# Windowed attention with both key blocks joined before the exponential, and changed places of splits and output copies

## What is computed

```python
# 1: attention, 8 heads of 64, window of 128, a bias per head that falls with the distance
scores = 0.125 * q @ k.T - slope[h] * abs(t - s)    # where 0 <= t - s < 128, else -1e9
x = softmax(scores) @ v
# 2: gated layer with a spatial product over tokens
h = relu(x @ w_in); u, v = h[..., :512], h[..., 512:]
v = (v - mean(v)) / sqrt(var(v) + 1e-6)
x = (u * (w_spatial @ v + b_spatial)) @ w_out
# 3: four experts, each a causal attention with one head of 64; a token takes the best two of w_gate
out = sum(weight[e] * (causal_softmax(0.125 * (x @ wq[e]) @ (x @ wk[e]).T) @ (x @ wv[e]) @ wo[e]))
```

## Time and profile before

| | |
|---|---|
| median of 3 runs | 510.14 us (510.04 to 512.35) |
| the profiled execution | 509.63 us, its span 507.8 us |
| granted TensorE clock | 0.999 |
| busy: PE, PEld, DVE, ACT, POOL | 97%, 84%, 59%, 54%, 39% |
| transposes of stage 1 (L1284) | 256 |

### The profile page before, as it was taken

One profiled execution on the slowest core, in us unless ns is written; L12 is line 12 of the kernel. 1 busy time (PEld: TensorE's weight loads), 2 busy tenths in 40 slices (PEclk: granted clock), 3 DMA queues, 4 the chain that ended last, 5 costly groups with the idle time before them and its releaser, 6 DMA issues.

```text
span 507.8 us, 10924 instructions
## 1 busy us (share of the span) xinstructions
PE 492.6 (97%) x3981; PEld 425.1 (84%) x3981; DVE 301.7 (59%) x1124; ACT 275.9 (54%) x828; POOL 200.4 (39%) x376
## 2 busy tenths in 40 slices
PE   8899999999999999999999999999999999999997
PEld 5677998998776789999876789999876779999875
DVE  6986773566766743246766762246777664235683
ACT  6876472446577643245567754235567663235554
POOL 4665432212434533433334553251244454161331
PEclk9999999999999999999999999999999999999999
DMA  7948020013110240004111070002301000000111
GB/s 216 326 109 254 3 83 1 1 36 106 43 53 2 61 127 1 1 1 113 50 32 43 2 188 1 1 1 48 114 24 53 1 3 1 1 0 13 36 43 52
DMA packets 31785, 28.51 MB, mean 56 GB/s; under 512 B 5810, under 2 KB 24242, under 8 KB 31732
## 3 DMA queue, kind: packets, MB, share of 16 engines
q1 hardware_dynamic: 31732, 27.82, 18.8%
HBM read 20.74 MB, written 4.72 MB: 50 GB/s over the span
## 4 chain that ended last, share of the span: by engine, by line
PE 74%; DVE 14%; ACT 5%; issue 3%; POOL 2%; DMA 1%; SPq 0%; DVEq 0%; ACTq 0%; POOLq 0%
PE bank L1254 14%; PE bank L1255 13%; PE bank L1256 13%; PE bank L1241 7%; PE bank L1284 6%; PE bank L1324 5%; PE bank L1515 4%; PE bank L1493 4%; PE bank L1475 4%; ACT p L748 2%; DVE neg L1039 2%; DVE k_lo L1141 1%; PE bank L1260 1%; DVE ring L857 1%; DVE q L1136 1%
## 5 line engine op out<-in xcount | busy, mean ns | idle before, releaser
L484 POOL TENSOR_SCALAR ring<-ring,r 128x256 f32<-128x256 f32 (+2 forms) x144 | 67.9, 483 | 83.0 <-DVE r L868 82.6
L567 POOL TENSOR_SCALAR p<-p,r,wgt 128x128 f32<-128x128 f32 (+3 forms) x64 | 38.1, 607 | 97.6 <-DVE wgt_last L1085 42.4
L589 ACT ACTIVATE ring<-ring,neg 128x256 f32<-128x256 f32 (+2 forms) x144 | 67.9, 474 | 13.9 <-DVE neg L857 13.7
L748 ACT ACTIVATE p<-bank,neg 128x128 f32<-128x128 f32 (+4 forms) x72 | 39.1, 547 | 47.0 <-DVE neg L1039 46.9
L857 DVE CUSTOM_DVE_ANT_0 ring<-bank,bias 128x256 f32<-128x256 f32 (+1 forms) x128 | 43.9, 385 | 16.5 <-PE bank L1241 16.1
L532 POOL TENSOR_TENSOR g_lo<-uT,g_hi 128x288 fp32r<-128x288 f32 x32 | 27.2, 872 | 42.6 <-ACT g_hi L710 42.6
L1284 PE MATMUL bank<-ident,ring 128*128 128x128 f32 (+1 forms) x256 | 37.8, 282 | 4.7 <-POOL ring L484 4.7
L1241 PE MATMUL bank<-k,q 64*128 64x256 f32 (+2 forms) x320 | 38.7, 369 | 1.2 <-DVE neg L857 0.8
L1324 PEld LDWEIGHTS bank<-pt,v_in 128*64 128x64 f32 x576 | 28.2, 136 | 13.6 <-issue 11.3
L1284 PEld LDWEIGHTS bank<-ident,ring 128*128 128x128 f32 (+1 forms) x256 | 26.9, 138 | 14.8 <-POOL ring L484 7.7
L1254 PE MATMUL bank<-g_hi,w_c_hi 128*128 128x288 f32 x128 | 38.5, 301 | 0.6
(11 more groups left out here) (184 smaller groups left out, 1402.5 us busy)
## 6 DMA issues: line engine op xcount, KB each, us to landing
v_in<-v SPq DMA_DIRECT2D x16, 256.0 KB, 4.0
out<-o_sb SPq DMA_DIRECT2D x16, 256.0 KB, 2.0
q<-qT SPq DMA_DIRECT2D x15, 256.0 KB, 4.7
k<-kT SPq DMA_DIRECT2D x15, 256.0 KB, 5.7
w_in_raw<-w_in SPq DMA_DIRECT2D x4, 512.0 KB, 6.5
w_cat_raw<-wcat SPq DMA_DIRECT2D x1, 1544.0 KB, 7.8
w_spatial_raw<-wsT SPq DMA_DIRECT2D x1, 1152.0 KB, 9.9
k_hi<-k_hi SPq DMA_DIRECT2D x8, 144.0 KB, 2.5
```

The source lines that it names most:

```text
L484: last = nc.gpsimd.tensor_scalar(p, p, r1[:, i % 2, h:h + 1], 0.0, ALU.mult, ALU.add)
L567: nc.gpsimd.tensor_scalar(p, p, r3[:, i % 2, e:e + 1], by, ALU.mult, ALU.mult).then_inc(s3_sd, 1)
L589: nc.scalar.activation(x, x, ACT.Exp, bias=neg1[:, u % SLOTS1:u % SLOTS1 + 1], scale=-1.0, accum_out=sum1[:, i % 2, h:h + 1]).then_inc(s1_ ...
L748: nc.scalar.activation(p3[:, w % P3_SLOTS, 0:n], scored3(w), ACT.Exp, bias=neg3[:, w % 4:w % 4 + 1], scale=1.0, accum_out=sum3[:, i % 2, e ...
```

## The change

For every query row, a key column of the query's own block is allowed exactly where the same column of the block before is masked. After bias and mask, DVE takes the smaller of both (`join1`: the ring holds the negated scores), so that 128 columns remain for the exponential, the scaling and one transpose per head. The transposed probabilities of all four heads are copied by ACT. DVE then multiplies this copy by `diag`, ones where the key is not behind the query. The values are `pt` times v of the block before, plus the masked `pt` times (v of the own block minus v of the block before). POOL makes these differences (`v_steps`), four per sequence. The first tile stays as it was. `norm_v` of the first three tiles goes from DVE to POOL, vn has a place for every tile, and its splits (`high_vn`, `low_vn`) move behind the turns.

In stage 3 `low_qk(5)` goes ahead of `top2_b(0)`, `low_qk(7)` ahead of the maxima of units 6 and 7, `high_qk(6)` ahead of two exponentials, and the output copies of tiles with index 1 and 2 ahead of the exponentials of their turn.

```diff
+def slots1(g):
+    at = units1(g)[0][0] % SLOTS1
+    return slice(at, at + len(units1(g)))
...
+vn = sb("vn", [P, NT, DM], F32, at + 4 * NT * DM)
...
+v_step = sb("v_minus_v_of_tile_above", [P, NT - 1, H, D], F32)
+diag = sb("keys_up_to_query", [P, P], F32)
...
+def joined1(b, g):
+    return (NG1 - 4) * b + g - 3
+def columns1(g):
+    return 2 * P if G1[g][0] < NT - 1 else P
+def t1_bank(g):
+    return 2 + (g % 2 if G1[g][0] == 0 else g // 2 % 2)
...
+    nc.gpsimd.affine_select(out=diag[:], in_=diag[:], compare_op=ALU.is_ge, fill=0.0, base=0,
+                            pattern=[[1, P]], channel_multiplier=-1).then_inc(s_diag, 1)
+    def v_steps(b, t):
+        pool.wait_ge(s_v_in[t - 1], 16 * (b + 1))
+        pool.wait_ge(s_v_in[t], 16 * (b + 1))
+        if t == NT - 1:
+            pool.wait_ge(s_vz if b else s_vz0, b if b else 1)
+        nc.gpsimd.tensor_tensor(v_step[:, t - 1], v_in[:, t], v_in[:, t - 1], ALU.subtract).then_inc(s_vd, 1)
...
-            p = ring[:, u % SLOTS1, 0:w]
+            p = ring[:, u % SLOTS1, 0:P]
...
+        def norm_v(i):
+            pool.wait_ge(s1_rs, NT * b + i + 1)
+            nc.gpsimd.tensor_scalar(vn[:, ORDER1[i], :], v_sb[:, i % 2, :], mv[:, i % 2, 0:1], rstd[:, i % 2, :],
+                                    ALU.subtract, ALU.mult).then_inc(s1_vn, 1)
...
+            if first and m % 2 and m // 2 + 1 < NT:
+                v_steps(0, m // 2 + 1)
             if first and m in TABLES_AT:
                 tables(TABLES_AT.index(m), 2 * m + 5)
             for i in range(NT - 2):
                 if m == 2 * i + 4 + first:
                     rstd_of(i)
-                if m == 2 * i + 6 + first:
-                    low_vn(i, 0)
-                    low_vn(i, 1)
+                    norm_v(i)
         pool.wait_ge(s1_xl, NT * (b + 1))
         nc.gpsimd.tensor_copy(xs[:, :, 0:LAST], x_hi[:, :, S - LAST:S])
         nc.gpsimd.tensor_copy(xs[:, :, LAST:P], x_lo[:, :, S - LAST:S]).then_inc(s1_xs, 1)
-        rstd_of(NT - 2)
-        for i in range(NT - 3, NT - 1):
+        for i in range(NT - 1):
             low_vn(i, 0)
             low_vn(i, 1)
+            if i == 0:
+                rstd_of(NT - 2)
...
-        for w in range(U3):
+        for w in range(2 * E):
             scale3(w)
         if more:
-            for g in range(3):
-                scale1(b + 1, g)
+            for t in range(1, NT - 1):
+                v_steps(b + 1, t)
+        for w in range(2 * E, U3):
+            scale3(w)
+        if more:
+            v_steps(b + 1, NT - 1)
+            scale1(b + 1, 0)
+            scale1(b + 1, 1)
+            scale1(b + 1, 2)
...
+        if i:
+            act.wait_ge(s1_cb, joined1(b, g))
         for u, h in units1(g):
-            x = ring[:, u % SLOTS1, 0:w]
-            act.wait_ge(s1_bi, U1 * b + u + 1)
+            x = ring[:, u % SLOTS1, 0:P]
+            if i == 0:
+                act.wait_ge(s1_bi, U1 * b + u + 1)
             nc.scalar.activation(x, x, ACT.Exp, bias=neg1[:, u % SLOTS1:u % SLOTS1 + 1], scale=-1.0,
                                  accum_out=sum1[:, i % 2, h:h + 1]).then_inc(s1_ex, 1)
...
-            qb, hs = ORDER1[m // 2], G1[2 * m][1]
-            act.wait_ge(s1_t, NG1 * b + 2 * m + 1)
+            n = (1 if m < 2 else 2) * columns1(2 * m)
+            act.wait_ge(s1_t, NG1 * b + 2 * m + (1 if m < 2 else 2))
             if m:
-                act.wait_ge(s1_pv, NG1 * b + 2 * m - 1)
-            for r, c0, c1 in regions(qb, keys1(qb), len(hs)):
-                last = nc.scalar.copy(pt[0:r, 0, c0:c1], bank[0:r, 2, c0:c1])
-            last.then_inc(s1_h, 1)
+                act.wait_ge(s1_pv, NG1 * b + 2 * m)
+            nc.scalar.copy(pt[:, 0, 0:n], bank[:, t1_bank(2 * m), 0:n]).then_inc(s1_h, 1)
...
+            if i < 3:
+                high_vn(i)
...
         high_qk(5)
+        high_qk(6)
         exp3(4)
         exp3(5)
-        high_qk(6)
         high_qk(7)
...
             copy_pt3(m)
+            for i in range(1, NT - 2):
+                if m == DEND3[i] + 2:
+                    copy_out(b, i)
             for w in units3(m):
                 exp3(w)
             if more and m >= ND3 - 3:
...
             if m == 1:
                 copy_out(b, 0)
                 exp_logits(1)
-            for i in range(1, NT - 1):
-                if m == DEND3[i] + 2:
-                    copy_out(b, i)
+            if m == DEND3[NT - 2] + 2:
+                copy_out(b, NT - 2)
...
+    def join1(b, g):
+        if g >= NG1 or G1[g][0] == 0:
+            return
+        n = P if G1[g][0] < NT - 1 else LAST
+        dve.wait_ge(s1_bi, U1 * b + units1(g)[-1][0] + 1)
+        x = ring[:, slots1(g), :]
+        nc.vector.tensor_tensor(x[:, :, 0:n], x[:, :, 0:n], x[:, :, P:P + n], ALU.min).then_inc(s1_cb, 1)
...
-            qb, hs = ORDER1[m // 2], G1[2 * m + 1][1]
-            dve.wait_ge(s1_t, NG1 * b + 2 * m + 2)
+            n = 2 * columns1(2 * m)
             if m:
                 dve.wait_ge(s1_pv, NG1 * b + 2 * m)
-            for r, c0, c1 in regions(qb, keys1(qb), len(hs)):
-                last = nc.vector.tensor_copy(pt[0:r, 1, c0:c1], bank[0:r, 3, c0:c1])
-            last.then_inc(s1_h2, 1)
+            if m < 2:
+                dve.wait_ge(s1_t, NG1 * b + 2 * m + 2)
+                nc.vector.tensor_copy(pt[:, 0, 2 * P:4 * P], bank[:, 3, 0:2 * P]).then_inc(s1_h2, 1)
+                return
+            if m == 2 and first:
+                dve.wait_ge(s_diag, 2)
+            dve.wait_ge(s1_h, ND1 * b + m + 1)
+            nc.vector.tensor_tensor(pt[:, 1, 0:n].rearrange("p (h r) -> p h r", h=4),
+                                    pt[:, 0, 0:n].rearrange("p (h r) -> p h r", h=4),
+                                    diag[:, 0:n // 4].unsqueeze(1).to_broadcast([P, 4, n // 4]), ALU.mult
+                                    ).then_inc(s1_h2, 1)
...
+            if m or first:
+                join1(b, 2 * m + 4)
             if not early:
                 copy_pt1_second(m)
             if 2 * m + 5 < NG1 and (m or first):
                 bias1(b, 2 * m + 5)
+                join1(b, 2 * m + 5)
...
-        top2_b(0)
         reciprocal3(1)
         low_qk(5)
+        top2_b(0)
         max3(4)
         max3(5)
         low_qk(6)
+        reciprocal3(2)
+        low_qk(7)
         max3(6)
         max3(7)
-        low_qk(7)
-        reciprocal3(2)
...
     def transpose1(b, g):
-        i = G1[g][0]
-        keys = keys1(ORDER1[i])
         pe.wait_ge(s1_sd, NG1 * b + g + 1)
+        at = columns1(g) * (g % 2) if G1[g][0] else 0
         for n, (u, h) in enumerate(units1(g)):
-            for j, kb in enumerate(keys):
-                k, c = rows(kb), P * (len(keys) * n + j)
-                last = nc.tensor.transpose(bank[0:k, 2 + g % 2, c:c + P], ring[:, u % SLOTS1, P * j:P * j + k], ident[:])
+            last = nc.tensor.transpose(bank[:, t1_bank(g), at + P * n:at + P * n + P], ring[:, u % SLOTS1, 0:P], ident[:])
         last.then_inc(s1_t, 1)
     def out_product(b, i, ks=(0, 1)):
...
     pe.wait_ge(s_tab, 1)
     def row(b, first, more):
-        def values1(g):
-            i, hs = G1[g]
+        def values1(m):
+            i = G1[2 * m][0]
             qb = ORDER1[i]
-            r, keys = rows(qb), keys1(qb)
-            if hs[0] == 0:
-                for t in keys:
-                    pe.wait_ge(s_v_in[t], 16 * (b + 1))
-                if i == NT - 1:
-                    pe.wait_ge(s_vz0 if first else s_vz, 1 if first else b)
+            r = rows(qb)
+            if m % 2 == 0:
+                pe.wait_ge(s_v_in[max(qb - 1, 0)], 16 * (b + 1))
+                if qb:
+                    pe.wait_ge(s_vd, (NT - 1) * b + qb)
                 if i >= 2:
                     pe.wait_ge(s1_xl, NT * b + i - 1)
-            if g % 2:
-                pe.wait_ge(s1_h2, ND1 * b + g // 2 + 1)
-            else:
-                pe.wait_ge(s1_h, ND1 * b + g // 2 + 1)
-            for kb in keys:
-                for j, h in enumerate(hs):
-                    c, at = place(qb, keys, len(hs), j, kb), r * (h // 2)
+            def product(g, values, part, start, stop):
+                for j, h in enumerate(G1[g][1]):
+                    at, c = r * (h // 2), columns1(g) * (g % 2) + r * j
                     last = nc.tensor.matmul(bank[D * (h % 2):D * (h % 2) + D, x_bank(i), at:at + r],
-                                            v_in[:, kb, h, :], pt[:, g % 2, c:c + r],
-                                            start=(kb == keys[0]), stop=(kb == keys[-1]))
-            last.then_inc(s1_pv, 1)
+                                            values[:, h, :], pt[:, part, c:c + r], start=start, stop=stop)
+                if stop:
+                    last.then_inc(s1_pv, 1)
+            pe.wait_ge(s1_h, ND1 * b + m + 1)
+            if qb == 0:
+                product(2 * m, v_in[:, 0], 0, True, True)
+                pe.wait_ge(s1_h2, ND1 * b + m + 1)
```

(10 more changed lines are left out.)

35 lines of the change are left out of this document (16 added, 19 removed).

## The result

The changed kernel took **518.59 us** (median, 517.53 to 520.22) where the kernel before took 510.24 beside it: a ratio of 1.016 (95% interval 1.012 to 1.020), slower by 1.6%. The forecast was 502.5 with a range of 495 to 509.5. It was wrong in sign and in size.

A forecast was written before the change was run, and what follows sets the result against it. The prediction took TensorE, busy 97% of the span, as the bound, with VectorE next. Its terms, -4.1 + 0.5 - 2.4 - 2.9 + 1.2 = -7.7 us from 509.63, led to 502.5 us against the median, range 495 to 509.5.

The forecast's parts named there:

- over 1.5 us of room: POOL in the turns: a late scaling would stall the next turn's transposes, but has this much slack.
- Stage 1 of sequences 1 to 3: Windowed attention: fewer transposes, partly offset by VectorE's added work; 1.4 us per sequence, -4.1 in all, bounds 0 and -9.1.
- the waits that I added: Pairs of turns: TensorE waits for VectorE's late mask product, so a pair takes 8.7 us instead of TensorE's 8.16.
- rival A: TensorE keeps its pace everywhere, with VectorE's waits in the turns vanishing: 494 us, chance 0.14.
- Sequence 0: First stage there: VectorE's added work cancels TensorE's saving and one v difference comes late; +0.5 us, bounds -3.0 and +5.
- Entry and output copies: Third stage: earlier splits at the causal entry give -2.4 us, output copies moved ahead give -2.9.
- Differences ahead of the ninth scaling: Sequences 1 to 3: three v differences on POOL delay a scaling, a new stall of 0.4 us; +1.2 in all.
- The low halves of vn: Moved together behind the turns, 1.43 us a tile, covered by TensorE's u and v products; no cost counted.
- Rival C: VectorE and POOL exclude each other in the turns, VectorE waiting out whole scalings: 522.5 us, chance 0.09.
- The chance of 0.10 on slower: Whole kernel: probability given to a measured time slower by more than 0.5%.
- something else of the moved work: Catch-all case that other moved work comes late, with no place or size named; chance 0.03.
- the surest sign of being wrong: TensorE waiting elsewhere, above all for POOL's scalings, would show the prediction wrong; no size given.

The follow-up runs named there:

- e1: Changed kernel with the normalisations of tiles 0 to 2 back on VectorE in the turns: 508.59 us, ratio 0.998.
- e7: Changed kernel with POOL's normalisations written as multiply-then-add, after a 128x1 operation that makes the shift: 512.15 us, ratio 1.005.
- e3: Changed kernel with normalisations back on VectorE and no differences of v (wrong attention values): 502.02 us, ratio 0.985.
- e12: As e10, with the mask product of turn 2 behind the first bias, reciprocal and join in sequences 1 to 3: 498.10 us, ratio 0.976.
- e11: As e9, with the join left out in the first stage of sequence 0 (attention wrong there): 500.49 us, ratio 0.981.
- e4: Kernel before the change with the third-stage edits alone (late splits and two output copies moved ahead): 503.98 us, ratio 0.989.
- e2: Changed kernel without the differences of v; the second product reads v itself (wrong attention values): 511.11 us, ratio 1.002.
- e10: As e9, but the first stage of sequence 0 computed as in the kernel before the change: 499.61 us, ratio 0.978.
- e9: As e1, with later sequences' v differences at the third stage's end, two before and two behind the next first scaling: 505.09 us, ratio 0.990.
- e8: Changed kernel with e7's normalisation, v differences moved (some into turns 1 and 3), turn 2's mask product behind the first bias: 510.29 us, ratio 1.000.

## Why the prediction was wrong

Between forecast and result lie 16 us. By the stretches 8.5 of them are in the first stage of sequence 0, 2.9 in the first stages of the others, 4.0 behind the spatial products, and 0.8 before the first values.

**The step that failed** is the sentence that POOL "has over 1.5 us of room", on which the normalisation was moved to POOL at no price. Its duration there was never bounded. The nearest rows had two prices for 512 columns on POOL: expert scalings at 0.77 and the two halves of vn_lo at 1.43. Neither was set down, and the true 2.3 is above both. No row stands beside the 1.5 of room either, and what counts is what stands in the queue ahead of a scaling in the turn in which it falls. e1 puts this step at 9 to 10 us: 4.8 in sequence 0 and 1.4 in each other. e7 splits it: some 6 are the slow form of the operation, and 3.6 its place in the queue.

**Stage 1 of sequences 1 to 3**, -4.1. Measured -1.2 with the change (50.58 to 50.2), and -5.3 in e1 and e3, where POOL is free of the normalisations. The forecast's prices for VectorE were good: joins run 0.32 to 0.35 from start to start, the mask product 0.61. But of the waits that I added, 0.54 a pair, hardly one came: a pair is 8.24 and near TensorE's own 8.16. That is rival A's pace. Against it stand the turns 0, 1 and 2 with their order of operations, which I had not looked at: turn 2 to 3 got 0.23 longer, because VectorE stood before the mask product, waiting for ScalarE's copy, with the bias behind it that frees TensorE's bank. e12 takes this out. A mask product and a bias behind it, in VectorE's timeline of sequence 1:

```profile
172.10 0.68 DVE L985 TENSOR_TENSOR pt<-pt,keys_up_to_query 128x512 f32<-128x512 f32 x1
172.70 0.42 DVE L904 CUSTOM_DVE_ANT_0 ring<-bank,bias 128x256 f32<-128x256 f32 x1
```

**Sequence 0**, +0.5 with bounds -3 and +5. Measured +9.0, outside the bounds: 4.8 for the normalisations (e1), 1.5 for the differences (e1 against e3), and the 2.7 left in e3, which I put down to VectorE because leaving out the joins alone gives 4.3 in e11. The forecast had VectorE at 22.9 of 22.8 us for five turns and called it even; from the values of turn 2 to those of turn 7 it was 22.8 before, 26.8 with the change and still 24.95 in e3. That I saw the bound and gave it nothing is the second fault of this forecast. A smaller slip: its own 17.4 less 16.69 is 0.7, not 0.8, and with the last tile's 0.43 back that makes +0.3, not +0.5.

**Entry and output copies**, -2.4 and -2.9. Right: 5.3 forecast, 5.5 in e4 (the second wait at the entry was 0.38 by its own two numbers, 0.97 less 0.59, and not 0.31). In the changed kernel the product at the causal entry follows without a gap, where the earlier trace rows had 0.36 from start to start:

```profile
240.52 0.22 PE L1548 MATMUL bank<-causalr,identr 128*128 128x128 f32 x1
240.57 0.35 PE L1317 MATMUL bank<-g_hi,w_c_hi 128*128 128x288 f32 x1
```

**Differences ahead of the ninth scaling**, +1.2, priced too low. Measured 1.6 to 1.9 a sequence, 5.2 in all (e2). The stall was 0.9 instead of 0.4, because POOL waited for two landings in turn, and the other half came through VectorE's small operations, which the step did not name.

**The low halves of vn**, moved together behind the turns and priced at nothing: right in sum. In e10 the first stage of sequence 0 is 0.86 shorter than before (51.60), and the stretch behind it 0.97 longer than in e4 (85.87 against 84.90), where TensorE waits once for ScalarE.

**Rival C** named the right pair of engines and the wrong loser. In the turns VectorE's operations with two SBUF sources did not lose; POOL's scalings beside them did, 1.34 for two instead of 0.72:

```profile
171.78 0.41 DVE L915 TENSOR_TENSOR ring<-ring 128x256 f32<-128x256 f32 x1
```
```profile
170.40 0.72 POOL L516 TENSOR_SCALAR ring<-ring,r 128x128 f32<-128x128 f32 x2 [0.93 <-DVE r L924]
171.95 1.34 POOL L516 TENSOR_SCALAR ring<-ring,r 128x128 f32<-128x128 f32 x2 [0.83 <-DVE r L924]
```

The second pair starts 0.17 behind a join, the first of these lines, and 0.15 before the mask product shown above, whose 0.68 is its common length. It ended at 173.29, 0.51 after that product. Beside a difference of 1.26 that was under way it is the other way round; the mask product, 0.68 in the turns, started at 18.17 in sequence 0 and took 1.25:

```profile
17.61 1.26 POOL L508 TENSOR_TENSOR v_minus_v_of_tile_above<-v_in 128x512 f32<-128x512 f32 x1
```
```profile
18.17 1.25 DVE L985 TENSOR_TENSOR pt<-pt,keys_up_to_query 128x512 f32<-128x512 f32 x1 [0.66 <-ACT pt L677]
```

The Trainium skill ("SBUF — State Buffer", Who interferes with whom) states that the order of issue decides who waits. The trace agrees where POOL's scaling started behind the join (0.6 us lost by POOL) and where the mask product started behind the difference (0.6 lost by VectorE). It does not show why the mask product at 172.10, which started behind the scaling, lost nothing. The forecast cited this order and did not follow it through: it looked only at scalings of 0.37 in POOL's queue, and not at its own new differences of 1.3, beside which VectorE lost 0.6 here and 0.8 in the third stage (1.02 instead of 0.18).

The chance of 0.10 on slower stood almost wholly on rival C. What came was part of the 0.03 left for "something else of the moved work". No rival was made for POOL's queue, though the text itself named a wait for POOL's scalings as the surest sign of being wrong.

## What to carry to other kernels

When work is moved to an engine that is busy 40% of the time, price each operation by a row of that engine with the same pair of operations (the two arithmetic steps of one instruction), and then look at what is queued behind it in that very turn: an idle share says nothing about a scaling of 0.37 us that has to be ready in time. A stage that has extra work in the first iteration (here the weights' splits) is another kernel; e10 keeps the old form there and the new one elsewhere, and that was worth 5.5 us over e9, beside it on the same chip. Add up a change that helps one stage and hurts another by stages, as the table of stretches does, before any theory is made.

## What was not expected of the hardware

- On POOL, subtract-then-multiply with two column operands took 2302 ns (2.07 to 2.70) for 128x512 in float32, multiply-then-add 829 (0.76 to 1.40 us) and multiply-multiply 772. On VectorE the same subtract-then-multiply takes 0.53.
- Operations of 128x1 on POOL took 0.19 to 0.90 us. The two ahead of a normalisation (0.19 and 0.56) cost its queue as much as two scalings of 128 columns (0.72).
- TensorE's granted clock, full all through sequence 0 before the change, was 0.66 between 20 and 25 us and 0.73 between 50 and 55 after it. The windows of the changed kernel:

```profile
15.00:20.00 5.00, 2.69 (x26) 1.64 (x26) 4.27 (x14) 2.60 (x10) 2.76 (x5) 1.00 1.14 291
20.00:25.00 5.00, 3.90 (x22) 2.75 (x18) 4.76 (x21) 3.12 (x11) 3.39 (x6) 0.66 0.92 336
...
50.00:55.00 5.00, 2.26 (x10) 2.13 (x10) 1.10 (x3) 0.37 (x1) 2.71 (x3) 0.73 0.15 13
```

  A part of each stretch ran at the lower of the two levels, 1.2 GHz, after TensorE had been busy only 2.69 of 5 us, or in the stall of 2.74. It is mostly a sign of the waits and not their cause. e2 and e3 are the same program up to turn 5; e3 had the dip (0.66) and e2 had not (1.00), and from values of turn 2 to those of turn 4 they took 11.43 and 11.06 us. The changed kernel and e7, alike up to there too, took 11.57 with the dip and 11.39 without. In e8 a run at a mean clock of 1.000 had a span of 508.4 and one at 0.993 had 508.7; in e9 two at 1.000 had 503.8 and 504.0, and two at 0.993 had 502.8 and 502.1. What the dip at 50 us cost alone was not measured.
